# A gated recurrence and a two-layer network on one core: a plain first stretch, sums kept in PSUM, and another order of the blocks

## The chip, the cores and the metric

One Trainium2 chip, one of its cores. The time is device microseconds of one execution. Three runs of the kernel before gave 1103.45, 1106.84 and 1106.91 us, median 1106.84.

## The reference

Two parts follow each other. A recurrence along time, per batch and channel, and then a two-layer network with a gate on each of the 12,160 tokens, 256 channels wide with 2048 hidden values:

```
sig = 1 / (1 + exp(-f_logit))                 # (2, 6080, 256)
f = lower_bound + (1 - lower_bound) * sig
h = f[t] * h + (1 - f[t]) * x[t]              # for t in 0..6079, kept as token t
u = h @ w_in                                  # 256 x 2048
g = u * clip(u + 3, 0, 6) / 6
y = g @ w_out                                 # 2048 x 256
```

All inputs and outputs are float32.

## The kernel before

**Precision.** Every matrix operand is split in two: a rounded part ("hi", float32r) and what is left ("lo"). A product is three matmuls: hi*hi, hi*lo, lo*hi (L566, L568, L570 for the first layer, L587 to L589 for the second). ScalarE makes each hi part by a copy that rounds, VectorE or POOL makes the lo part by a subtraction.

**Tiles.** The 6080 time steps of each of the two batches are cut into a first span of 960 and five of 1024, which gives 12 tiles (t = 0 to 11; `TILES`), batches in turn. Within a tile, tokens are dealt in runs of four into two halves, FIRST and SECOND, so that a matmul has 480 columns in tiles 0 and 1 and 512 in the others.

**Seven products.** The first layer is a 2x2 block multiplication done with seven products instead of eight (Strassen's scheme in Winograd's form). Its operands are sums of quarters of the weights (`sum_w7`, POOL, once for each of the 8 blocks of 256 hidden values) and sums of quarters of the state (t_a, t_b, t_c; POOL, once per tile). The results are put together through running sums in a PSUM bank: `x_ps` takes A11, then S2, S1 and S4 on top of it, and between them ScalarE copies the state of the bank to `h_sb` (`copy_p1` L311, `copy_p16` L317, `copy_p165` L321). VectorE adds those copies to `z_ps` or `v_ps`: C11 (`add_c11`, L461), C22 (`add_c22`, L467), C21 (`add_c21`, L473). C12 is `x_ps` itself. C11, C22 and C21 are written to `h_sb`.

**A block** (q counts them, 96 in all; j is its number in the tile) has 7 products and 8 second-layer products ("downs", two for each of the four results), 45 matmuls. The downs are those of block q-1 and lie between the products of block q. For each result C: clip on ScalarE (`clip_lower`, L332), gate on VectorE (`gate_h`, L479), rounding on ScalarE (`round_g`, L339), rest on VectorE (`rest_of_g`, g_lo, L484), then the two downs.

**State of the next tile** is made during a tile: sigmoid on ScalarE (L282, blocks 2 and 3), then on VectorE drive (L426) and gate of the state (L432, a multiply and add with one input), and two scans (L440, L443), in blocks 2 to 5, always in front of the C11 sum; POOL and ScalarE then make the seven operands.

**Order.** Each engine has one queue, written out by hand, and runs it in order; the engines meet on semaphores. TensorE's order is in the loop at L600, ScalarE's at L363, VectorE's at L520, POOL's at L250, and SyncE issues all DMAs (L172 to L200). Before the first block, TensorE runs 36 small matmuls that only keep it busy, while VectorE, ScalarE and POOL make the state, operands and weights of block 0.

## Time and profile before

| What the page shows | |
|---|---|
| profiled execution | 1102.24 us, its span 1100.5 us |
| TensorE (PE) busy | 1018.1 us, 93% |
| VectorE (DVE) busy | 861.7 us, 78% |
| ScalarE (ACT) busy | 739.8 us, 67% |
| GpSimd (POOL) busy | 232.0 us, 21% |
| chain that ended last | DVE 35%, PE 30%, ACT 18%, issue 13% |
| L339 rounding, L332 clip of h_sb, mean | 617 ns, 720 ns |
| L317 copy of x_ps, mean | 584 ns |
| L479 gate, L484 g_lo, mean | 801 ns, 700 ns |
| L227 operand rest on POOL, mean | 1545 ns |
| x load of 512 KB, issue to landing | 7.1 us |
| mean granted clock of TensorE | 0.977 of full |

Busy time of TensorE counts overlapping matmuls once; a matmul's row lasts longer than the distance to the next one. So the rate is read from starts, and what is lost from the distance between equal places of two blocks or tiles. Idle time on an engine counts only where TensorE ends up waiting for it.

### The profile page before, as it was taken

The page shows a single profiled execution, that of the slowest core. Times are in us where ns is not written, and L with a number is a line of the kernel's source. Part 1 is how long each engine was busy: PE and PEld are TensorE (multiplying, and loading weights), DVE is VectorE, ACT ScalarE, POOL GpSimd, SP SyncE. Part 2 cuts the span into 40 slices and gives each one's busy share as a digit, 9 for nine tenths or more (in the row PEclk, how much of TensorE's full clock was granted, in tenths as well). Part 3 has the DMA queues.
Part 4 walks back from the last instruction along what each step waited for, and adds up shares of the span by engine and source line. Part 5 has one row for each costly group of instructions (what it writes and reads, how often), then busy time and mean ns, then how long its engine had stood idle before and what let it go on. Part 6 is the DMA issues. An engine that isn't in the chain of part 4 may idle for free.

```text
span 1100.5 us, 12941 instructions
## 1 busy us (share of the span) xinstructions
PE 1018.1 (93%) x4356; PEld 823.4 (75%) x4356; DVE 861.7 (78%) x1190; ACT 739.8 (67%) x1229; POOL 232.0 (21%) x176
## 2 busy tenths in 40 slices
PE   2788999998999999999899899999999999989998
PEld 2566787887777787787777778777778778777886
DVE  7687779788779778768778868877977886887675
ACT  3666676776776677676677677577767667766765
POOL 5655402202201301311210220220130121022000
PEclk7899999999999999999999999999999999999999
DMA  6200030030030030011003003003002000200000
GB/s 224 72 1 1 1 113 1 1 113 1 1 116 1 1 115 1 0 42 74 1 1 115 1 0 115 1 1 115 1 1 94 22 1 13 103 1 1 39 1 39
DMA packets 12707, 42.39 MB, mean 39 GB/s; under 512 B 1376, under 2 KB 1376, under 8 KB 12640
## 3 DMA queue, kind: packets, MB, share of 16 engines
q1 hardware_dynamic: 12640, 41.56, 10.4%
q8 instruction: 35, 0.57, 0.2%
q14 instruction: 32, 0.26, 0.1%
HBM read 29.10 MB, written 12.45 MB: 38 GB/s over the span
## 4 chain that ended last, share of the span: by engine, by line
DVE 35%; PE 30%; ACT 18%; issue 13%; DMA 2%; POOL 1%; SPq 0%; ACTq 0%; DVEq 0%; POOLq 0%
DVE g L479 14%; DVE g_lo L484 9%; ACT g_hi L339 8%; ACT g L332 6%; PE y_ps L587 5%; PE y_ps L588 5%; PE y_ps L589 5%; DVE h_sb L461 5%; PE x_ps L566 3%; PE x_ps L568 3%; PE x_ps L570 3%; DVE x_sb L426 3%; DVE x_sb L440 3%; DMA x_sb<-in_x 2%; PE v_ps L566 2%
## 5 line engine op out<-in xcount | busy, mean ns | idle before, releaser
L339 ACT CAST g_hi<-g 128x512 fp32r<-128x512 f32 (+1 forms) x384 | 233.9, 617 | 147.8 <-DVE g L479 146.3
L479 DVE SCALAR_TENSOR_TENSOR g<-g,h_sb 128x512 f32<-128x512 f32 (+1 forms) x288 | 230.6, 801 | 101.0 <-ACT g L332 99.0
L587 PE MATMUL y_ps<-g_hi,w_out_hi 128*128 128x512 f32 (+1 forms) x768 | 300.2, 391 | 0.3 <-DVE g_lo L484 0.3
L588 PE MATMUL y_ps<-g_lo,w_out_hi 128*128 128x512 f32 (+1 forms) x768 | 300.2, 391 | 0.0
L589 PE MATMUL y_ps<-g_hi,w_out_lo 128*128 128x512 f32 (+1 forms) x768 | 299.7, 390 | 0.0
L332 ACT ACTIVATE g<-h_sb,half 128x512 f32<-128x512 f32 (+1 forms) x288 | 207.4, 720 | 128.0 <-DVE h_sb L461 126.4
L484 DVE TENSOR_TENSOR g_lo<-g,g_hi 128x512 fp32r<-128x512 f32 (+1 forms) x384 | 261.2, 700 | 38.6 <-ACT g_hi L339 15.0
L566 PE MATMUL x_ps<-op_hi,w_hi 128*128 128x512 f32 (+1 forms) x384 | 154.2, 402 | 36.8 <-ACT h_sb L311 25.0
L587 PEld LDWEIGHTS y_ps<-g_hi,w_out_hi 128*128 128x128 f32 x768 | 145.5, 190 | 30.7 <-DVE g_lo L484 0.8
L589 PEld LDWEIGHTS y_ps<-g_hi,w_out_lo 128*128 128x128 f32 x768 | 145.7, 190 | 29.5
L588 PEld LDWEIGHTS y_ps<-g_lo,w_out_hi 128*128 128x128 f32 x768 | 145.5, 189 | 29.6
L568 PE MATMUL x_ps<-op_lo,w_hi 128*128 128x512 f32 (+1 forms) x384 | 151.3, 394 | 0.0
L570 PE MATMUL x_ps<-op_hi,w_lo 128*128 128x512 f32 (+1 forms) x384 | 150.6, 392 | 0.0
L566 PEld LDWEIGHTS x_ps<-op_hi,w_hi 128*128 128x128 f32 x384 | 73.6, 192 | 60.7 <-ACT h_sb L311 33.3
L566 PE MATMUL v_ps<-op_hi,w_hi 128*128 128x512 f32 (+1 forms) x192 | 81.8, 426 | 40.0 <-DVE h_sb L467 39.4
L461 DVE TENSOR_TENSOR h_sb<-z_ps,h_sb 128x512 f32<-128x512 f32 (+1 forms) x96 | 64.9, 676 | 66.3 <-PE z_ps L570 66.3
L236 POOL TENSOR_TENSOR t_a<-x_sb 128x512 f32<-128x512 f32 (+1 forms) x12 | 16.1, 1338 | 362.9 <-DVE x_sb L443 362.9
L317 ACT COPY h_sb<-x_ps 128x512 f32<-128x512 f32 (+1 forms) x96 | 56.0, 584 | 47.8 <-PE x_ps L570 47.5
L566 PEld LDWEIGHTS v_ps<-op_hi,w_hi 128*128 128x128 f32 x192 | 36.7, 191 | 67.6 <-DVE h_sb L467 62.2
L570 PEld LDWEIGHTS x_ps<-op_hi,w_lo 128*128 128x128 f32 x384 | 73.7, 192 | 15.1
L568 PEld LDWEIGHTS x_ps<-op_lo,w_hi 128*128 128x128 f32 x384 | 73.8, 192 | 14.1
L227 POOL TENSOR_TENSOR op_lo<-x_sb,op_hi 128x512 fp32r<-128x512 f32 (+1 forms) x34 | 52.1, 1545 | 148.7 <-ACT op_hi L307 148.7
(64 smaller groups left out, 1202.1 us busy)
## 6 DMA issues: line engine op xcount, KB each, us to landing
z_sb<-in_z SPq DMA_DIRECT2D x20, 512.0 KB, 6.2
x_sb<-in_x SPq DMA_DIRECT2D x20, 512.0 KB, 7.1
out_y<-y_sb SPq DMA_DIRECT2D x9, 1024.0 KB, 5.3
w_raw<-in_w_in SPq DMA_DIRECT2D x8, 256.0 KB, 7.5
w_out_raw<-in_w_out SPq DMA_DIRECT2D x8, 256.0 KB, 7.5
z_sb<-in_z SPq DMA_DIRECT2D x4, 480.0 KB, 4.4
x_sb<-in_x SPq DMA_DIRECT2D x4, 480.0 KB, 5.6
out_y<-y_sb SPq DMA_DIRECT2D x2, 960.0 KB, 5.3
```

Source lines behind the costliest of these rows:

```text
L317: nc.scalar.copy(h_sb[:, C21, 0:n], x_ps[:, q % 2, 0:n]).then_inc(p16_copied, 1)
L332: nc.scalar.activation(g[:, u, 0:n], h, ACT.Relu, bias=half[:], scale=1.0 / 6.0).then_inc(clipped_ready[u], 1)
L339: nc.scalar.copy(g_hi[:, u, 0:n], g[:, u, 0:n]).then_inc(g_hi_ready[u], 1)
L461: nc.vector.tensor_tensor(h_sb[:, C11, 0:n], z_ps[:, 0:n], h_sb[:, C11, 0:n], ALU.add).then_inc(h_ready[C11], 1)
L479: nc.vector.scalar_tensor_tensor(g[:, u, 0:n], g[:, u, 0:n], 1.0, h, ALU.min, ALU.mult).then_inc(g_ready[u], 1)
L484: nc.vector.tensor_tensor(g_lo[:, u, 0:n], g[:, u, 0:n], g_hi[:, u, 0:n].bitcast(F32), ALU.subtract).then_inc(g_lo_ready[u], 1)
L566: nc.tensor.matmul(out[:, 0:n], w7_hi[:, j, o], op_hi[:, b, o, 0:n], start=start, stop=False, skip_group_check=True)
L568: nc.tensor.matmul(out[:, 0:n], w7_hi[:, j, o], op_lo[:, b, o, 0:n], start=False, stop=False, skip_group_check=True)
L570: return nc.tensor.matmul(out[:, 0:n], w7_lo[:, j, o], op_hi[:, b, o, 0:n], start=False, stop=True, skip_group_check=True)
L587: nc.tensor.matmul(out, w_out_hi[:, f, at], g_hi[:, u, 0:n], start=opens, stop=False)
L588: nc.tensor.matmul(out, w_out_hi[:, f, at], g_lo[:, u, 0:n], start=False, stop=False)
L589: return nc.tensor.matmul(out, w_out_lo[:, f, at], g_hi[:, u, 0:n], start=False, stop=closes)
```

## The change

It has three parts.

**1. The first 960 tokens (batch 0) are worked plainly,** with the weights as they are, not with seven products. This "head" is in two parts of 448 and 512 tokens, 16 units of 128 hidden values each (32 units, v = 0 to 31). A unit is two first-layer products and two downs, 12 matmuls; four units are in flight (`LEAD`), in the four banks `x_ps` (2), `z_ps`, `v_ps`. The clip and the gate read the bank directly. Only 11 seven-product tiles are left (88 blocks), of which the first has 480 columns. The plain weights are rounded and their rests made one block at a time in the head's units; the sums for the seven products are made on POOL in three groups during the head (`sum_weights`, `make_s3`), S3's last, since its place holds a weight that the head still reads. State and operands of tile 0 are made in units 13 to 31. Warm-up matmuls: 28 instead of 36.

**2. Sums in place.** C11 is added into `z_ps` and C21 into `v_ps`; clip and gate read them there. C22 stays in `h_sb`.

**3. A new order in the blocks.** TensorE: both C22 downs before S1; S4 between the C21 downs, in front of A22. ScalarE: C12 is clipped before C21, and roundings of C12 and C21 move behind the next block's `copy_p1`. VectorE: the next tile's work stands behind the last gate of a block; rest_of_g for C21 and C12 moves around the next C11 sum. The gate of the state moves from VectorE to ScalarE (`make_gate`, an ACTIVATE with scale and bias). Scans for channel half 0 come in blocks 0 and 1, for half 1 in blocks 3 and 4, one per block; drives in blocks 7 and 2. SyncE loads z as soon as the scan has read it, two tiles ahead, and x when its sums are made.

```diff
-WARM_UP = 36
+WARM_UP = 28
+LEAD = 4
...
-    TILES = STEPS * B
+    TILES = STEPS * B - 1
+    HEAD_AT = (0, FIRST_SPAN - N)
+    HEAD_N = (FIRST_SPAN - N, N)
+    HEAD = len(HEAD_N) * F
+    GROUPS = (slice(0, 2), slice(2, 5), slice(5, 8))
...
 @block.gpsimd
+            def make_s3(i):
+                at = GROUPS[i]
+                raw = raw_of(at)
+                pool.wait_ge(head_up_done, F + 2 * at.stop)
+                nc.gpsimd.tensor_tensor(w7_raw[:, at, S3_T3], raw[:, :, 0], raw[:, :, 2],
+                                        ALU.subtract).then_inc(w_s3_ready, 1)
...
 @block.scalar
+            def make_gate(t, k):
+                n = 2 * half_span(t)
+                act.wait_ge(drive_ready[k], t + 1)
+                nc.scalar.activation(z_sb[:, k, 0:n], z_sb[:, k, 0:n], ACT.Identity, bias=one[:],
+                                     scale=lb_minus_one[:, k:k + 1]).then_inc(gate_ready[k], 1)
...
+            def head_clip(v):
+                s, n = v % LEAD, HEAD_N[v // F]
+                act.wait_ge(head_up_done, v + 1)
+                if v >= LEAD:
+                    act.wait_ge(head_g_lo_ready, v - LEAD + 1)
+                nc.scalar.activation(g[:, s, 0:n], head_bank(s, n), ACT.Relu, bias=half[:],
+                                     scale=1.0 / 6.0).then_inc(head_clipped_ready, 1)
...
 @block.vector
             def add_c11(q, n):
-                nc.vector.tensor_tensor(h_sb[:, C11, 0:n], z_ps[:, 0:n], h_sb[:, C11, 0:n],
+                nc.vector.tensor_tensor(z_ps[:, 0:n], z_ps[:, 0:n], h_sb[:, C11, 0:n],
                                         ALU.add).then_inc(h_ready[C11], 1)
...
             def add_c21(q, n):
-                nc.vector.tensor_tensor(h_sb[:, C21, 0:n], v_ps[:, 0:n], h_sb[:, C21, 0:n],
+                nc.vector.tensor_tensor(v_ps[:, 0:n], v_ps[:, 0:n], h_sb[:, C21, 0:n],
                                         ALU.add).then_inc(h_ready[C21], 1)
...
 @block.tensor
+            for v in range(LEAD, HEAD):
+                for d in range(K):
+                    head_down(v - LEAD, d)
+                for k in range(K):
+                    up = head_up(v, k)
+                up.then_inc(head_up_done, 1)
...
                 product(q, A12_B21, z_ps, True, n).then_inc(p2_ready, 1)
-                if q > 0:
-                    down(q - 1, C22, 0)
+                before(q, C22, 0)
+                before(q, C22, 1)
                 pe.wait_ge(p16_copied, q + 1)
                 product(q, S1_T1, bank, False, n).then_inc(p165_ready, 1)
-                if q > 0:
-                    pe.wait_ge(h_ready[C21], q)
+                if q == 0:
+                    pe.wait_ge(head_g_ready, HEAD)
+                else:
+                    pe.wait_ge(g_ready[C21], q)
                 product(q, S3_T3, v_ps, True, n).then_inc(p7_ready, 1)
-                if q > 0:
-                    down(q - 1, C22, 1).then_inc(down_done[C22], 1)
-                    down(q - 1, C21, 0)
+                before(q, C21, 0)
+                pe.wait_ge(p165_copied, q + 1)
+                product(q, S4_B22, bank, False, n).then_inc(c12_ready, 1)
+                before(q, C21, 1)
                 pe.wait_ge(h_ready[C22], q + 1)
                 product(q, A22_T4, v_ps, False, n).then_inc(p74_ready, 1)
```

TensorE's queue of a middle tile, before: from the end of product S3 (the first row) to product A22. The numbers in the semaphores' names are 0 for C11, 1 for C22, 2 for C21, 3 for C12.

```order
L570 MATMUL v_ps<-op_hi,w7_lo 128x512
L587 MATMUL y_ps<-g_hi,w_out_hi 128x512 [waits g_lo_ready1]
L588 MATMUL y_ps<-g_lo,w_out_hi 128x512
L589 MATMUL y_ps<-g_hi,w_out_lo 128x512
L587 MATMUL y_ps<-g_hi,w_out_hi 128x512 [waits g_lo_ready2]
L588 MATMUL y_ps<-g_lo,w_out_hi 128x512
L589 MATMUL y_ps<-g_hi,w_out_lo 128x512
L566 MATMUL v_ps<-op_hi,w7_hi 128x512 [waits h_ready1]
L568 MATMUL v_ps<-op_lo,w7_hi 128x512
L570 MATMUL v_ps<-op_hi,w7_lo 128x512
```

After, from the same place:

```order
L931 MATMUL v_ps<-op_hi_odd,w7_lo 128x512
L947 MATMUL y_ps<-g_hi,w_out_hi 128x512 [waits g_lo_ready2]
L948 MATMUL y_ps<-g_lo,w_out_hi 128x512
L949 MATMUL y_ps<-g_hi,w_out_lo 128x512
L929 MATMUL x_ps<-op_hi_odd_top,w7_hi 128x512 [waits p165_copied]
L930 MATMUL x_ps<-op_lo_odd_top,w7_hi 128x512
L931 MATMUL x_ps<-op_hi_odd_top,w7_lo 128x512
L947 MATMUL y_ps<-g_hi,w_out_hi 128x512 [waits g_lo_ready2]
L948 MATMUL y_ps<-g_lo,w_out_hi 128x512
L949 MATMUL y_ps<-g_hi,w_out_lo 128x512
L929 MATMUL v_ps<-op_hi_odd,w7_hi 128x512 [waits h_ready1]
```

S4 (x_ps) and a second C21 down now stand where a C22 down stood, so three products lie between S3 and the wait for the C22 sum (h_ready1), where two did.

VectorE's queue of a middle tile, before: blocks 4 and 5 begin with the work for the next tile, in front of the C11 sum (L461).

```order
L426 SCALAR_TENSOR_TENSOR x_sb<-z_sb,one_minus_lb,x_sb 128x1024 [waits x_loaded1,sig_ready1]
L432 TENSOR_SCALAR z_sb<-z_sb,lb_minus_one 128x1024 [waits drive_ready1]
L461 TENSOR_TENSOR h_sb<-z_ps,h_sb 128x512 [waits p1_copied,p2_ready]
L479 SCALAR_TENSOR_TENSOR g<-g,h_sb 128x512 [waits clipped_ready0]
L467 TENSOR_TENSOR h_sb<-v_ps,h_sb 128x512 [waits p165_copied,p7_ready]
L484 TENSOR_TENSOR g_lo<-g,g_hi 128x512 [waits g_hi_ready0]
L479 SCALAR_TENSOR_TENSOR g<-g,h_sb 128x512 [waits clipped_ready1]
L473 TENSOR_TENSOR h_sb<-v_ps,h_sb 128x512 [waits p16_copied,p74_ready]
```

After, from the last gate of a block (L727 with v_ps), a scan, and the begin of the next:

```order
L727 SCALAR_TENSOR_TENSOR g<-g,v_ps 128x512 [waits clipped_ready2]
L699 SCALAR_TENSOR_TENSOR x_sb<-z_sb,carry,x_sb 128x512 [waits carry_ready,gate_ready0]
L732 TENSOR_TENSOR g_lo<-g,g_hi 128x512 [waits g_hi_ready2]
L710 TENSOR_TENSOR z_ps<-z_ps,h_sb 128x512 [waits p1_copied,p2_ready]
L732 TENSOR_TENSOR g_lo<-g,g_hi 128x512 [waits g_hi_ready3]
L727 SCALAR_TENSOR_TENSOR g<-g,z_ps 128x512 [waits clipped_ready0]
L716 TENSOR_TENSOR h_sb<-v_ps,h_sb 128x512 [waits p165_copied,p7_ready]
L732 TENSOR_TENSOR g_lo<-g,g_hi 128x512 [waits g_hi_ready0]
L727 SCALAR_TENSOR_TENSOR g<-g,h_sb 128x512 [waits clipped_ready1]
```

The scan (L699) stands behind the gates. The subtractions g_lo (L732) of the block before lie on both sides of the C11 sum (L710), which now writes z_ps. The state's gate (L432) has left this queue.

ScalarE's queue, before: end of block 0 of a tile, begin of block 1. L346 copies y of the tile before.

```order
L332 ACTIVATE g<-h_sb,half 128x512 [waits g_lo_ready1,h_ready1]
L339 CAST g_hi<-g 128x512 [waits down_done1,g_ready1]
L346 COPY y_sb<-y_ps 128x128x4 [waits y_stored,down_done2] x2
L332 ACTIVATE g<-h_sb,half 128x512 [waits g_lo_ready2,h_ready2]
L332 ACTIVATE g<-x_ps,half 128x512 [waits g_lo_ready3,c12_ready]
L311 COPY h_sb<-x_ps 128x512 [waits p1_ready]
L346 COPY y_sb<-y_ps 128x128x4 [waits y_stored,down_done3]
L339 CAST g_hi<-g 128x512 [waits down_done2,g_ready2]
L339 CAST g_hi<-g 128x512 [waits down_done3,g_ready3]
L317 COPY h_sb<-x_ps 128x512 [waits g_ready2,p16_ready]
L346 COPY y_sb<-y_ps 128x128x4 [waits y_stored,down_done3]
```

After:

```order
L473 ACTIVATE z_sb<-z_sb,one,lb_minus_one 128x1024 [waits drive_ready0]
L518 COPY y_sb<-y_ps 128x128x4 [waits y_stored,down_done2]
L499 ACTIVATE g<-x_ps,half 128x512 [waits g_lo_ready3,c12_ready]
L508 CAST g_hi<-g 128x512 [waits down_done1,g_ready1]
L518 COPY y_sb<-y_ps 128x128x4 [waits y_stored,down_done2]
L499 ACTIVATE g<-v_ps,half 128x512 [waits g_lo_ready2,h_ready2]
L478 COPY h_sb<-x_ps 128x512 [waits p1_ready]
L508 CAST g_hi<-g 128x512 [waits down_done3,g_ready3]
L508 CAST g_hi<-g 128x512 [waits down_done2,g_ready2]
L518 COPY y_sb<-y_ps 128x128x4 [waits y_stored,down_done3]
L484 COPY h_sb<-x_ps 128x512 [waits h_ready2,p16_ready]
L518 COPY y_sb<-y_ps 128x128x4 [waits y_stored,down_done3]
```

Between the clip of C22 and the clip of C21 (v_ps) of block 0 there are now the state's gate and two y copies, and in block 1 the two roundings stand in front of the y copy that waits for down_done3.

## Rows read from the trace of the kernel before

**Rows 1.** Busy time by window; columns: window, its length, each engine, clock, DMA
```profile
0.00:28.00 28.00, 8.20 (x39) 7.27 (x39) 20.62 (x23) 9.82 (x14) 16.66 (x18) 0.73 0.62 220
28.00:130.10 102.10, 84.06 (x342) 67.95 (x342) 78.98 (x97) 63.65 (x110) 60.92 (x49) 0.92 0.06 20
130.10:212.80 82.70, 79.63 (x362) 67.03 (x360) 66.56 (x99) 58.49 (x103) 16.34 (x11) 1.00 0.11 38
212.80:1009.80 797.00, 760.29 (x3241) 610.90 (x3240) 636.39 (x883) 549.98 (x910) 138.05 (x99) 0.99 0.10 36
```

**Rows 2.** Timeline, last tile, TensorE; columns: start us, length us, engine, line, operation
```profile
1069.75 0.39 PE L566 MATMUL x_ps<-op_hi,w_hi 128*128 128x512 f32 x1
...
1079.95 0.39 PE L566 MATMUL x_ps<-op_hi,w_hi 128*128 128x512 f32 x1
```

**Rows 3.** Timeline, TensorE, 480 columns
```profile
35.08 0.38 PE L566 MATMUL x_ps<-op_hi,w_hi 128*128 128x480 f32 x1
...
35.73 0.38 PE L566 MATMUL x_ps<-op_hi,w_hi 128*128 128x480 f32 x1
```

**Rows 4.** Timeline, ScalarE: the first copy of tiles 1, 2 and 11
```profile
130.15 0.55 ACT L311 COPY h_sb<-x_ps 128x480 f32<-128x480 f32 x1
...
212.75 0.58 ACT L311 COPY h_sb<-x_ps 128x512 f32<-128x512 f32 x1
...
1009.82 0.58 ACT L311 COPY h_sb<-x_ps 128x512 f32<-128x512 f32 x1
```

**Rows 5.** Waits from 212.8 to 1009.8; columns: us in total, times, longest
```profile
PEld v_ps L566 <- DVE h_sb L467: 52.6, 45, 2.6
```

**Rows 6.** Timeline, VectorE, blocks 4 and 5 of a middle tile
```profile
608.87 1.28 DVE L426 SCALAR_TENSOR_TENSOR x_sb<-z_sb,one_minus_lb,x_sb 128x1024 f32<-128x1024 f32 x1
610.19 1.66 DVE L432 TENSOR_SCALAR z_sb<-z_sb,lb_minus_one 128x1024 f32<-128x1024 f32 x1
611.77 0.68 DVE L461 TENSOR_TENSOR h_sb<-z_ps,h_sb 128x512 f32<-128x512 f32 x1
613.24 0.69 DVE L479 SCALAR_TENSOR_TENSOR g<-g,h_sb 128x512 f32<-128x512 f32 x1 [0.79 <-ACT g L332]
613.85 0.68 DVE L467 TENSOR_TENSOR h_sb<-v_ps,h_sb 128x512 f32<-128x512 f32 x1
...
621.32 2.13 DVE L443 TENSOR_TENSOR_SCAN x_sb<-z_sb,x_sb 128x512 f32<-128x512 f32 x1
623.37 0.66 DVE L461 TENSOR_TENSOR h_sb<-z_ps,h_sb 128x512 f32<-128x512 f32 x1
624.82 1.77 DVE L479 SCALAR_TENSOR_TENSOR g<-g,h_sb 128x512 f32<-128x512 f32 x1 [0.79 <-ACT g L332]
```

**Rows 7.** Timeline, TensorE and ScalarE, the same blocks
```profile
609.49 0.39 PE L570 MATMUL x_ps<-op_hi,w_lo 128*128 128x512 f32 x1
...
609.91 0.59 ACT L317 COPY h_sb<-x_ps 128x512 f32<-128x512 f32 x1 [0.68 <-PE x_ps L570]
...
614.59 0.50 PE L566 MATMUL v_ps<-op_hi,w_hi 128*128 128x512 f32 x1 [0.63 <-DVE h_sb L467]
```

**Rows 8.** Timeline, POOL, the same tile
```profile
624.77 1.27 POOL L265 TENSOR_TENSOR t_c<-x_sb 128x512 f32<-128x512 f32 x1
```

**Rows 9.** Groups, 212.8 to 1009.8; columns: count, busy us, mean ns, idle before
```profile
L479 DVE SCALAR_TENSOR_TENSOR g<-g,h_sb 128x512 f32<-128x512 f32 x216 | 170.7, 790 | 71.5 <-ACT g L332 69.9
...
L479 DVE SCALAR_TENSOR_TENSOR g<-g,x_ps 128x512 f32<-128x512 f32 x72 | 49.0, 681 | 4.8 <-ACT g L332 4.8
...
L282 ACT ACTIVATE z_sb<-z_sb 128x1024 f32<-128x1024 f32 x18 | 19.1, 1061 | 0.0
```

**Rows 10.** Timeline, the start: first sigmoid, first drive, second product
```profile
4.36 1.00 ACT L282 ACTIVATE z_sb<-z_sb 128x960 f32<-128x960 f32 x1 [2.34 <-DMA z_sb<-in_z]
...
7.09 1.22 DVE L426 SCALAR_TENSOR_TENSOR x_sb<-z_sb,one_minus_lb,x_sb 128x960 f32<-128x960 f32 x1 [2.31 <-DMA x_sb<-in_x]
...
28.63 0.77 PE L566 MATMUL x_ps<-op_hi,w_hi 128*128 128x480 f32 x1 [8.35 <-ACT h_sb L311]
```

807 lines of the change are left out of this document (561 added, 246 removed).

## The prediction

> **What bounds the kernel now.** I read the stages first [rows 1]. TensorE is busy for 95 or 96% of both windows between 130 and 1010 us, so the reader should see a kernel near its matmul rate, with a poor start and a small leak everywhere else. How fast it could go stands in the last tile, which prepares no next tile: two starts of the first product of a block lie 1079.95 - 1069.75 = 10.20 us apart, 45 matmuls of 512 columns at 0.2267 us each [rows 2]. At 480 columns three matmuls take 35.73 - 35.08 = 0.65 us, so one is 0.2167 and a block 9.75 us [rows 3]. (A row's own duration, 0.39, overlaps its neighbours; starts count.)
>
> Against that rate the stages lose this. The copy that follows the first product of a tile marks the tiles [rows 4]. Up to 130.15 us one tile is done whose matmuls need 78.0: 52 us lost. Tile 1 takes 82.6 for 78.0. From 212.75 to 1009.82 nine tiles take 797.1 us, 88.56 each, against 8 x 10.20 = 81.6: 63 us lost. Of the waits in that stretch the weight load in front of the second v_ps product is the large one, 52.6 us over 45 waits, always for the C22 sum on VectorE (L467) [rows 5].
>
> Why that sum is late is in VectorE's order of time [rows 6]. From the C11 sum (611.77) to the C11 gate (613.24) pass 1.47 us, because ScalarE's clip lies between; the C22 sum starts 0.61 later, and TensorE starts its product right at its end, 614.59, after 0.63 us idle [rows 7]. In front of the C11 sum stand drives, gates and scans. A second effect sits in the same rows: the scan took 2.13 and a gate with both inputs in SBUF 1.77, while a sum with a PSUM input in the same neighbourhood took 0.66. POOL was working then [rows 8]. Over the stretch the gate with h_sb averages 790 ns, the one with x_ps 681 [rows 9].
>
> [...]
>
> **Steady tiles, step by step.** I put a block's time zero at its first product and each product at 0.68 us (3 x 0.2267). Order now: A11 0, C11 downs, S2 2.04, A12 2.72, C22 downs, S1 4.76, S3 5.44, C21 down, S4 6.80, C21 down, A22 8.16, C12 downs, end 10.20. A result can be read 0.42 us after its last matmul starts (609.49 to 609.91) [rows 7], so z_ps at 3.6, v_ps after S3 at 6.3.
> - C22 sum: before, its consumer A22 came 1.36 us after S3, now 2.04 after it, and S3 itself comes 0.68 later after A12. From the C11 sum's start to the C22 sum's end pass at least 1.47 + 0.61 + 0.68 = 2.76 us. Before, A22 wanted it 3.2 after z_ps: 0.4 us room. Now it wants it at 8.16, 4.56 after z_ps: 1.8 us room, 1.2 once v_ps decides (6.3 + 0.68).
> - The new tight place is S4 behind copy_p165, which is queued on ScalarE behind the C11 clip: sum 3.6 to 4.3, clip to 5.0, copy to 6.2, wanted 6.80. The sum may be 1.2 us late.
> - VectorE's load per block [rows 6, 9]: 3 sums at 0.68, 4 gates at 0.68, 4 g_lo at 0.69 (the small table has 0.70 as the mean over all), plus per tile two drives and four scans at 1.28 (the two gate instructions, 1.66 beside POOL, leave): 7.5 + 0.96 = 8.5 us of 10.20. At most one 1.28 piece falls into one block, and behind the last gate; before it was two (608.87 to 611.77) in front of the C11 sum [rows 6]. Lateness is made good within the block.
> - The C11, C21 and head gates now read PSUM, so they fall to 0.68 even beside POOL. The two sums written into PSUM have no row. Lower bound: 0.66, the shortest sum. Upper bound: the longest row of rows 6 at 512 columns but the scan, 1.77. I take 0.68, the row it is nearest to (same instruction, same inputs).
> - ScalarE per block (the small table's means): 3 copies at 0.58, 4 roundings at 0.62, clips at 0.67 from PSUM: 6.95; per tile 2 sigmoids and now 2 gates at 1.06, 7 operand roundings, 4 y copies: 1.37 per block, 8.3 together. The gate on ScalarE has no row; it is the same ACTIVATE at the same 1024 columns as the sigmoid, 1.06 [rows 9]; bounds 0.72, the mean clip of half the columns, and twice that, 1.45 (0.8 us more per tile, 8 in all).
> - Where ScalarE is too full: block 0 of a tile, gate and two y copies between clip C22 and clip C21. Clip C21 ends near 12.0 instead of 10.6, so the next copy_p1 ends at 12.5 and S2 wants it at 12.24; then two roundings stand in front of the y copy for the SECOND half, C22's first down waits for it 0.3, its second 0.4. Loss about 1.3 us per tile. Queued behind: everything on ScalarE, but the blocks 2 to 7 have room. I add 0.3 per tile for scans beside POOL.
> - SyncE's queue: z is now loaded as soon as the state is scanned, x once POOL has made t_c (near block 6), and the y store stands behind both. x lands 7.1 us after its issue (small table), the drive comes at the end of block 7, some 10 us later: nothing, and if the cover went, one drive late by the difference, absorbed as above.
> So a tile takes 81.6 + 1.6 = 83.2 (bounds 81.8 and 86.0), nine of them 748.8 against 797.1.
>
> **The head.** It has 384 matmuls for 960 tokens, 24 more than the 360 of the seven-product way: 192 of 448 columns (0.203 each, an estimate on the line through rows 2 and 3) and 192 of 512 (0.2267).
> - Start: z and x come in 448 columns instead of 960. Before, the sigmoid starts at 4.36 and the drive at 7.09 [rows 10]; the drive should now start near 5.3. Drive 0.6, gate 0.4, scan 1.2, w_lo 0.7, operand rest 0.6: first product near 9 us. The second channel, with scans as long as the 2.13 of 621.32 [rows 6], gives 13 to 14; clip, gate, rounding and g_lo of the first unit let the first down start near 17. The kernel before reaches its second product at 28.63 [rows 10].
> - From there 336 matmuls up to the first seven-product block (four units' downs lie in that block): 168 x 0.203 + 168 x 0.2267 = 72.2, to 89.
> - Is TensorE the slowest there? Per unit it needs 2.4 to 2.7 us. VectorE: gate and g_lo 1.3, 32 units 42; g_lo beside POOL 0.35 more (estimate between 0 and 1.08), 11; five w_lo, head gates, scans and the next tile's state work 18: 71 us in 72. It is level. From a product's end to its down 7.1 us pass and the chain needs 5, so 2 us of lateness are hidden. ScalarE waits in its queue for POOL's weight sums and t_c near the end; clips behind it are 1 to 3 us late. I charge 6 us for all this and for a TensorE at the lower clock after the idle start (a mean of 0.73 in the first window [rows 1], which lies between the two levels, 2.4 GHz and half of it): first block at 95.
> - Eight warm-up matmuls fewer, all of them over before 9 us either way: nothing.
> - The weights' sums are hidden: S3's sum waits for the head's products up to unit 20, is needed at 100.
> - First seven-product tile: 8 x 9.75 + 1.4 = 79.4, so 1920 tokens are done at 174.4. Before it was 212.75 - 0.87 = 211.9. Gain 37.5.
>
> **Sum.** 174.4 + 748.8 = 923.2. The last tile and its tail took 1100.5 - 1008.95 = 91.55; I add the 1.3 of the tile boundary and 1.4 because g_lo of C21, wanted second by the last downs, is now made last: 94.3. Span 1017.5. The profiled execution was 1102.24 for a span of 1100.5, so 1019.2; the median of the runs lay 0.4% over the profiled one, of which I take half: 1021 us.
>
> **Rivals.**
> - Steady tiles stay held by ScalarE: its queue gains two gates, and if every block, not only block 0, loses 0.55 us, a tile takes 86.0: 28 us more, 1049. For it: 8.3 of 10.2 busy and in-order waits. Against it: no other block has three extra pieces, and the clips wait less than before (L332 for L461 loses a scan in front).
> - The head is held by VectorE: if each of 32 g_lo pays the full 1.08, it has 94 us of work for 72, less what POOL's pauses and the charged 6 give back: 14 more, 1035. [...]
> - No boundary loss and a clean head: 16 + 5 less, 1000.
> - Slower: the sums written in place. Two per block, 88 blocks. VectorE has 10.2 - 8.5 = 1.7 us room, less 0.3 for POOL; once a sum costs more than 0.7 extra, VectorE sets the block, and each further 0.1 us costs 17.6 us. 86 us are eaten at 0.7 + 0.49 = 1.2 us extra, a sum of 1.88 us instead of 0.68. At 2.0 us the time is 1128. Against it: no 512-column row is that long, and PSUM reads are not dear.
> The Trainium skill, "VectorE: DVE Perf Modes", section The TRN2 errata, gives VectorE 120 fixed cycles from PSUM against 58 from SBUF, 65 ns more; the trace disagrees (681 ns with x_ps [rows 9], 0.69 with h_sb where POOL rested, at 613.24 [rows 6]). Even doubled in both sums it would be an estimate of 0.26 us per block, inside the room.
> - The change not doing what it says: the order of instructions shows the new order on TensorE and the gates on ScalarE, so none.
>
> **From this the numbers.** Forecast (1002 to 1035) 0.68, ScalarE 0.12, VectorE in the head 0.10, clean 0.05, in-place sums dear 0.05, of which 0.04 slower and 0.01 even. A difference within 0.3% can't be told from none. Low 1000, high 1052.
>
> **What would show it.** Right: blocks of 10.2 us in tiles 1 to 9 save for the first two; the wait of v_ps on L716 nearly gone; the sums L710 and L722 at 0.68; first head product near 9 us, first seven-product block near 95. Wrong: L710 over 1.0 us; S4 waiting for copy_p165 in every block; gaps of TensorE behind g_lo in the head of over 0.5 us per unit.

## The result, and the profile after

The changed kernel takes 1013.84 us, the median of 4 runs (1013.15 to 1014.54), beside 1105.14 us, the median of 4 runs of the kernel before on the same chip. The ratio is 0.9176, 95% interval 0.9152 to 0.92. The forecast was 1021 us in a range of 1000 to 1052. The profiled execution took 1013.79 us, its span 1011.6.

The chain that ended last, by engine. Before, its shares were 35% on VectorE and 30% on TensorE.

```profile
PE 87%; DVE 4%; issue 3%; ACT 3%; POOL 1%; DMA 0%; SPq 0%; ACTq 0%; DVEq 0%; POOLq 0%
```

Busy time by window after the change, for [rows 1] (columns as there). The windows are: the start, the head's first units, the rest of the head, the first seven-product tile, the nine middle tiles, the last tile. The bounds at 96.40, 175.50 and 918.30 lie 0.9 us before the copies that mark the tiles.

```profile
0.00:17.00 17.00, 12.74 (x52) 10.99 (x52) 9.37 (x17) 7.39 (x13) 4.21 (x7) 0.90 0.88 296
17.00:42.50 25.50, 24.45 (x120) 21.99 (x119) 24.44 (x34) 18.26 (x33) 10.84 (x6) 1.00 0.29 97
42.50:96.40 53.90, 51.76 (x229) 42.33 (x227) 44.92 (x50) 37.03 (x61) 40.66 (x28) 1.00 0.18 60
96.40:175.50 79.10, 77.06 (x351) 65.62 (x352) 64.61 (x95) 58.02 (x103) 20.66 (x14) 1.00 0.11 34
175.50:918.30 742.80, 741.33 (x3241) 606.11 (x3240) 602.66 (x865) 550.54 (x926) 144.94 (x99) 1.00 0.11 36
918.30:1011.60 93.30, 87.66 (x385) 71.74 (x383) 60.30 (x93) 58.82 (x99) 0.00 (x0) 0.99 0.06 23
```

TensorE is busy for 741.3 of 742.8 us in the middle tiles, where it was 760.3 of 797.0 [rows 1]. The copy that marks the tiles [rows 4] is now L478 (timeline, ScalarE; the first copies of the first and second seven-product tile and of the last):

```profile
97.32 0.56 ACT L478 COPY h_sb<-x_ps 128x480 f32<-128x480 f32 x1
...
176.42 0.59 ACT L478 COPY h_sb<-x_ps 128x512 f32<-128x512 f32 x1 [0.64 <-PE x_ps L931]
...
919.21 0.59 ACT L478 COPY h_sb<-x_ps 128x512 f32<-128x512 f32 x1 [0.30 <-PE x_ps L931]
```

So 1920 tokens are done 36.3 us earlier (212.75 - 176.42). The nine middle tiles take 742.8 us for 797.1, 82.5 each for 88.6: 54.3 us less. The last tile with its tail is 1.8 us longer. Together 88.8, which is the difference of the spans, 1100.5 - 1011.6 = 88.9.

The waits of TensorE's weight loads from 177 to 918 us, for [rows 5]:

```profile
PEld y_ps L947 <- ACT y_sb L518: 6.6, 18, 0.5
PEld x_ps L929 <- ACT h_sb L478: 5.2, 9, 0.6
```

The wait for the C22 sum, 52.6 us before, is gone. What is left comes at the boundary of each tile: one wait for `copy_p1` and two for the y copies. The groups of VectorE in the whole page of the profile (columns: count, busy us, mean ns, idle before), for [rows 9]:

```profile
L716 DVE TENSOR_TENSOR h_sb<-v_ps,h_sb 128x512 f32<-128x512 f32 (+1 forms) x88 | 60.5, 688 | 43.4 <-PE v_ps L931 43.2
...
L710 DVE TENSOR_TENSOR z_ps<-z_ps,h_sb 128x512 f32<-128x512 f32 (+1 forms) x88 | 60.9, 693 | 17.0 <-PE z_ps L931 17.0
...
L727 DVE SCALAR_TENSOR_TENSOR g<-g,v_ps 128x512 f32<-128x512 f32 (+1 forms) x88 | 60.2, 684 | 14.7 <-ACT g L499 14.7
L727 DVE SCALAR_TENSOR_TENSOR g<-g,h_sb 128x512 f32<-128x512 f32 (+1 forms) x88 | 60.5, 687 | 11.7 <-ACT g L499 11.0
```

A sum written into PSUM costs 693 ns, one written into SBUF 688. The gates with h_sb no longer average 790 ns: three of the four gates read PSUM, and the fourth (C22, with h_sb) now falls where POOL rests, in 87 of its 88 instances.

### The profile page after: what moved, and what is told of

Its sections match the earlier page's. It is cut to its first block, busy times and chain, and to the rows that moved or that the text cites. A ratio compares the mean times of both kernels' runs of the same rounds, so it can differ in the third digit from the quotient of the medians.

```text
span 1011.6 us, 12907 instructions
## 1 busy us (share of the span) xinstructions
PE 995.0 (98%) x4372; PEld 818.8 (81%) x4372; DVE 806.3 (80%) x1149; ACT 730.1 (72%) x1230; POOL 221.3 (22%) x154
## 4 chain that ended last, share of the span: by engine, by line
PE 87%; DVE 4%; issue 3%; ACT 3%; POOL 1%; DMA 0%; SPq 0%; ACTq 0%; DVEq 0%; POOLq 0%
PE y_ps L947 15%; PE y_ps L948 14%; PE y_ps L949 14%; PE x_ps L929 8%; PE x_ps L930 7%; PE x_ps L931 7%; PE v_ps L931 4%; PE v_ps L930 4%; PE v_ps L929 4%; PE z_ps L929 2%; PE z_ps L930 2%; PE z_ps L931 2%; PE y_ps L911 1%; PE y_ps L913 1%; PE y_ps L912 1%
## 5 line engine op out<-in xcount | busy, mean ns | idle before, releaser
L732 DVE TENSOR_TENSOR g_lo<-g,g_hi 128x512 fp32r<-128x512 f32 (+1 forms) x352 | 271.1, 770 | 42.1 <-ACT g_hi L508 41.3
L508 ACT CAST g_hi<-g 128x512 fp32r<-128x512 f32 (+1 forms) x352 | 209.1, 620 | 14.4 <-DVE g L727 13.7
L499 ACT ACTIVATE g<-v_ps,half 128x512 f32<-128x512 f32 (+1 forms) x88 | 60.5, 687 | 58.3 <-DVE v_ps L722 58.3
L499 ACT ACTIVATE g<-z_ps,half 128x512 f32<-128x512 f32 (+1 forms) x88 | 60.4, 687 | 57.5 <-DVE z_ps L710 56.3
L716 DVE TENSOR_TENSOR h_sb<-v_ps,h_sb 128x512 f32<-128x512 f32 (+1 forms) x88 | 60.5, 688 | 43.4 <-PE v_ps L931 43.2
L727 DVE SCALAR_TENSOR_TENSOR g<-g,x_ps 128x512 f32<-128x512 f32 (+1 forms) x88 | 59.8, 680 | 40.1 <-ACT g L499 40.1
L499 ACT ACTIVATE g<-h_sb,half 128x512 f32<-128x512 f32 (+1 forms) x88 | 63.6, 723 | 24.0 <-DVE h_sb L716 23.7
L929 PE MATMUL x_ps<-op_hi_even,w_hi 128*128 128x512 f32 (+1 forms) x192 | 75.2, 391 | 2.7 <-ACT h_sb L478 2.3
L710 DVE TENSOR_TENSOR z_ps<-z_ps,h_sb 128x512 f32<-128x512 f32 (+1 forms) x88 | 60.9, 693 | 17.0 <-PE z_ps L931 17.0
L930 PE MATMUL x_ps<-op_lo_even,w_hi 128*128 128x512 f32 (+1 forms) x192 | 74.5, 388 | 0.0
L931 PE MATMUL x_ps<-op_hi_even,w_lo 128*128 128x512 f32 (+1 forms) x192 | 74.4, 388 | 0.0
L727 DVE SCALAR_TENSOR_TENSOR g<-g,v_ps 128x512 f32<-128x512 f32 (+1 forms) x88 | 60.2, 684 | 14.7 <-ACT g L499 14.7
L727 DVE SCALAR_TENSOR_TENSOR g<-g,h_sb 128x512 f32<-128x512 f32 (+1 forms) x88 | 60.5, 687 | 11.7 <-ACT g L499 11.0
L478 ACT COPY h_sb<-x_ps 128x512 f32<-128x512 f32 (+1 forms) x88 | 51.2, 581 | 25.7 <-PE x_ps L931 25.7
```

The source lines that it names most:

```text
L499: nc.scalar.activation(g[:, u, 0:n], up_result(q, u, n), ACT.Relu, bias=half[:], scale=1.0 / 6.0).then_inc(clipped_ready[u], 1)
L508: nc.scalar.copy(g_hi[:, u, 0:n], g[:, u, 0:n]).then_inc(g_hi_ready[u], 1)
L710: nc.vector.tensor_tensor(z_ps[:, 0:n], z_ps[:, 0:n], h_sb[:, C11, 0:n], ALU.add).then_inc(h_ready[C11], 1)
L716: nc.vector.tensor_tensor(h_sb[:, C22, 0:n], v_ps[:, 0:n], h_sb[:, C22, 0:n], ALU.add).then_inc(h_ready[C22], 1)
L727: nc.vector.scalar_tensor_tensor(g[:, u, 0:n], g[:, u, 0:n], 1.0, up_result(q, u, n), ALU.min, ALU.mult).then_inc(g_ready[u], 1)
L732: nc.vector.tensor_tensor(g_lo[:, u, 0:n], g[:, u, 0:n], g_hi[:, u, 0:n].bitcast(F32), ALU.subtract).then_inc(g_lo_ready[u], 1)
```

## The experiments

The trace says where the time went, not which part of the change brought it. Two parts aim at the same wait: the new order gives the C22 sum more room, and the sums in place keep the work in front of it short. All times are medians of 4 runs. They come from different chips, so the ratio, to the kernel before on the same chip, is the safer number to compare. "A tile" is the mean of the nine middle tiles between the marks above, from the one traced execution of each kernel; for the kernel before it is 88.56 us.

| Kernel | us | ratio, 95% interval | a tile, us |
|---|---|---|---|
| changed kernel | 1013.84 | 0.9176 [0.9152, 0.9200] | 82.53 |
| e1_sums_sbuf | 1017.08 | 0.9219 [0.9196, 0.9242] | 82.71 |
| e2_gate_dve | 1010.97 | 0.9165 [0.9143, 0.9186] | 81.68 |
| e3_pe_order | 1135.55 | 1.0297 [1.0267, 1.0327] | 90.80 |
| e4_pe_order_back | 1004.79 | 0.9111 [0.9089, 0.9133] | 81.59 |
| h1_sbuf_old_order | 1026.81 | 0.9300 [0.9286, 0.9314] | 83.69 |
| h2_in_place | 1063.34 | 0.9631 [0.9615, 0.9647] | 85.04 |
| h3_in_place_gate | 1064.90 | 0.9644 [0.9626, 0.9661] | 85.22 |
| g1_paired | 1005.11 | 0.9103 [0.9087, 0.9119] | 81.65 |
| g2_round_end | 1012.21 | 0.9170 [0.9150, 0.9190] | 82.55 |
| g4_all_back | 1035.70 | 0.9385 [0.9366, 0.9404] | 84.53 |
| g3_no_head | 1036.53 | 0.9390 [0.9371, 0.9410] | 82.52 |
| h4_best | 1003.68 | 0.9095 [0.9079, 0.9110] | 81.59 |

**e1_sums_sbuf: the sums out of PSUM again.** Changed kernel, and:

```diff
-                nc.vector.tensor_tensor(z_ps[:, 0:n], z_ps[:, 0:n], h_sb[:, C11, 0:n],
+                nc.vector.tensor_tensor(h_sb[:, C11, 0:n], z_ps[:, 0:n], h_sb[:, C11, 0:n],
...
-                nc.vector.tensor_tensor(v_ps[:, 0:n], v_ps[:, 0:n], h_sb[:, C21, 0:n],
+                nc.vector.tensor_tensor(h_sb[:, C21, 0:n], v_ps[:, 0:n], h_sb[:, C21, 0:n],
```

> The changed kernel with one part undone: the C11 and C21 sums go to SBUF (h_sb) again, and their gates read them there, so they have two SBUF inputs. Theory (room in the order carries the gain): the gates beside POOL cost up to 1.08 us more, 0.11 us on average over all, but 1.2 us of room take nearly all of it: 1014 to 1019 us, the gate L727 with h_sb near 0.79 mean, hardly a new wait on TensorE. Rival (sums in place are what removed the stalls): two contended gates per tile put about 1 us each on the path of ten tiles: 1032 us or more.

The time rose by 3.2 us, and the two intervals just touch. In the traces 1.8 us of the difference stand there before the first seven-product block has begun (its first copy at 99.16 for 97.32), where this edit changes nothing: TensorE was granted 0.84 of its clock in the first 17 us, where the changed kernel had 0.90. The middle tiles lose 0.18 us each, 1.6 in all. The gates with h_sb are slow again (VectorE's group of all three results that stand in SBUF, 177 to 910 us), yet TensorE waits 0.3 us in all for the C22 sum:

```profile
L723 DVE SCALAR_TENSOR_TENSOR g<-g,h_sb 128x512 f32<-128x512 f32 (+1 forms) x212 | 172.9, 815 | 27.7 <-ACT g L495 25.9
```

In the new order the sums in place are worth 2 to 3 us.

**e3_pe_order: TensorE's new order alone.** Kernel before, and in TensorE's loop:

```diff
-                    down(q - 1, C22, 0)
+                    down_both(q - 1, C22)
...
-                    down(q - 1, C22, 1).then_inc(down_done[C22], 1)
                     down(q - 1, C21, 0)
+                pe.wait_ge(p165_copied, q + 1)
+                product(q, S4_B22, bank, False, n).then_inc(c12_ready, 1)
+                if q > 0:
+                    down(q - 1, C21, 1).then_inc(down_done[C21], 1)
                 pe.wait_ge(h_ready[C22], q + 1)
                 product(q, A22_T4, v_ps, False, n).then_inc(p74_ready, 1)
-                if q > 0:
-                    down(q - 1, C21, 1).then_inc(down_done[C21], 1)
-                pe.wait_ge(p165_copied, q + 1)
-                product(q, S4_B22, bank, False, n).then_inc(c12_ready, 1)
```

> The kernel before with TensorE's new order alone (both C22 downs before S1, S4 and a C21 down between S3 and A22); ScalarE, VectorE and POOL as before. Theory (TensorE's order is the larger part of the steady gain): the wait for the C22 sum goes from 53 us to under 10, some comes back at C12 and C21, whose clips are in the old order; a tile falls from 88.6 to about 85.5, 1070 to 1080 us. Rival (what stands in front of the C11 sum on VectorE decides, the order only shifts who waits): 1095 or more.

It is 3% slower, where 1070 to 1080 us were expected. The waits of the weight loads from 212 to 1000 us:

```profile
PEld x_ps L566 <- ACT h_sb L311: 71.2, 60, 1.8
...
PEld v_ps L566 <- DVE h_sb L467: 5.7, 8, 0.7
```

The order does what I had computed for the C22 sum: 52.6 us of waiting become 5.7. But 71 us of another wait come in. The last tile, where no state work disturbs, shows the chain (timeline of VectorE, ScalarE, TensorE in turn):

```profile
1108.72 0.69 DVE L473 TENSOR_TENSOR h_sb<-v_ps,h_sb 128x512 f32<-128x512 f32 x1 [0.54 <-PE v_ps L570]
...
1109.44 0.72 ACT L332 ACTIVATE g<-h_sb,half 128x512 f32<-128x512 f32 x1 [0.61 <-DVE h_sb L473]
1110.07 0.67 ACT L332 ACTIVATE g<-x_ps,half 128x512 f32<-128x512 f32 x1
1110.93 1.22 ACT L339 CAST g_hi<-g 128x512 fp32r<-128x512 f32 x2 [0.18 <-DVE g L479]
1112.05 0.58 ACT L311 COPY h_sb<-x_ps 128x512 f32<-128x512 f32 x1
...
1112.68 0.50 PE L566 MATMUL x_ps<-op_hi,w_hi 128*128 128x512 f32 x1 [0.60 <-ACT h_sb L311]
```

A22 now ends later, so does the C21 sum. ScalarE, in its old order, clips C21 and C12 and rounds both before it copies the bank that S2 of the next block wants. Blocks 0 and 1 of a tile take 21.5 us together, and from block 2 on every block takes at least 11.09 us, in the last tile too, instead of 10.20. The changed kernel moves the roundings behind the copy, so it does not pay this; but the direction of the debt is shown: what the order gives the C22 sum it takes from the chain C21, ScalarE, `copy_p1`. The time lies where the rival had it (1095 or more), but that rival named VectorE's work in front of the C11 sum, and the wait that came in is one for ScalarE.

**e4_pe_order_back: everything but the order.** Changed kernel with the old order of products (shown), and C12's clip, gate and rounding behind C21's as before; the roundings stay behind `copy_p1`:

```diff
                 before(q, C22, 0)
-                before(q, C22, 1)
...
+                before(q, C22, 1)
                 before(q, C21, 0)
-                pe.wait_ge(p165_copied, q + 1)
-                product(q, S4_B22, bank, False, n).then_inc(c12_ready, 1)
-                before(q, C21, 1)
                 pe.wait_ge(h_ready[C22], q + 1)
                 product(q, A22_T4, v_ps, False, n).then_inc(p74_ready, 1)
+                before(q, C21, 1)
+                pe.wait_ge(p165_copied, q + 1)
+                product(q, S4_B22, bank, False, n).then_inc(c12_ready, 1)
```

> The changed kernel with the old order of products on TensorE (A22 before S4, one C22 down between S3 and it), and ScalarE's and VectorE's order of C12 and C21 turned back to match; head, sums in place and one piece of state work per block stay. Theory: room for the C22 sum falls to 0.4 us, every block with a drive or scan in front of it stalls 0.3 to 1 us: 3 us per tile, 1040 to 1050. Rival (order does not matter once VectorE has one piece per block): 1014 to 1020.

It is 9 us faster than the changed kernel (7 by the ratios, 8.5 in the middle tiles of the traces), below both the theory's range and the rival's. Between 175 and 910 us TensorE is never idle (busy time by window), and seven of the nine middle tiles are exactly 8 x 10.200 us:

```profile
175.00:910.00 735.00, 735.00 (x3245) 608.59 (x3243) 606.52 (x865) 552.49 (x925) 141.03 (x99) 1.00 0.11 36
```

The copy that is late in the changed kernel, the one of block 1 behind a tile's first block, is now in time: ScalarE reaches it 0.20 us before the product is done (timeline, ScalarE):

```profile
512.32 0.59 ACT L478 COPY h_sb<-x_ps 128x512 f32<-128x512 f32 x1 [0.20 <-PE x_ps L931]
```

My theory that the new product order is a main step of the gain falls here. In this kernel it is a loss. The edit takes the order of C12 and C21 on ScalarE and VectorE back with the products; the three were not separated.

**h1_sbuf_old_order: old order and sums in SBUF.** The kernel of e4 with the edit of e1.

> The changed kernel with the old order of products and of copies (as in e4_pe_order_back, 1004.79 us), and the sums of C11 and C21 written to SBUF again, nothing else. Theory: in the old order the sums in place are what carries the blocks, because with them the gates read PSUM and do not meet GpSimd's work; with the sums in SBUF the contended gates return and the matmuls of blocks 2, 5, 6 and 7 wait some 0.65 us each, 2.6 us per middle tile, nine tiles and a part of the last: 1025 to 1032 us. In the new order the same undoing cost 3.2 us. Rival: the old order has room enough by itself, since the state's gate is off VectorE: 1005 to 1010 us.

1026.81 us, 22 more than e4, as the theory had it. Middle tiles are 10.20 in blocks 0 to 4 and 11.03, 10.82 and 10.86 in blocks 5 to 7. The second row of the timeline (VectorE, then TensorE) is the C11 gate, 1.75 us with both inputs in SBUF beside POOL; the C22 sum stands behind it, and TensorE behind that:

```profile
566.66 0.69 DVE L706 TENSOR_TENSOR h_sb<-z_ps,h_sb 128x512 f32<-128x512 f32 x1
...
568.15 1.75 DVE L723 SCALAR_TENSOR_TENSOR g<-g,h_sb 128x512 f32<-128x512 f32 x1
569.83 0.68 DVE L712 TENSOR_TENSOR h_sb<-v_ps,h_sb 128x512 f32<-128x512 f32 x1
...
570.56 0.50 PE L925 MATMUL v_ps<-op_hi_odd,w_hi 128*128 128x512 f32 x1 [0.53 <-DVE h_sb L712]
```

POOL's work beside that gate:

```profile
566.16 3.19 POOL L352 TENSOR_TENSOR op_lo_even<-x_sb,op_hi_even 128x512 fp32r<-128x512 f32 x2 [0.20 <-ACT op_hi_even L464]
```

With e1 and e4 this closes a square. Old order: 1026.8 with the sums in SBUF, 1004.8 with the sums in place. New order: 1017.1 and 1013.8. Each of the two parts is a remedy for the same wait. The order gains 9.7 us where the sums are in SBUF and loses 9.1 where they are in place. The middle tiles of the traces say the same without the differences between chips and starts: 83.69 and 81.59 us in the old order, 82.71 and 82.53 in the new one.

**h2_in_place: the sums in place alone.** Kernel before with this part only (the clip and the gate read the bank; S3 waits for the gate of C21 in place of its sum):

```diff
-                nc.vector.tensor_tensor(h_sb[:, C11, 0:n], z_ps[:, 0:n], h_sb[:, C11, 0:n],
+                nc.vector.tensor_tensor(z_ps[:, 0:n], z_ps[:, 0:n], h_sb[:, C11, 0:n],
...
-                nc.vector.tensor_tensor(h_sb[:, C21, 0:n], v_ps[:, 0:n], h_sb[:, C21, 0:n],
+                nc.vector.tensor_tensor(v_ps[:, 0:n], v_ps[:, 0:n], h_sb[:, C21, 0:n],
...
-                    pe.wait_ge(h_ready[C21], q)
+                    pe.wait_ge(g_ready[C21], q)
```

> The kernel before with the sums of C11 and C21 left in place in PSUM, nothing else of the change. Theory: the sums in place alone take most of the stalls out of the blocks, some 3.5 us of the 5.9 to 7.3 us by which a tile of before is above its matmuls; ten tiles: 1065 to 1080 us. The blocks in which VectorE also holds the state's gate and drive keep a stall. Rival: the state's gate on VectorE and the order of TensorE set the stalls, and the sums alone give under 1 us per tile: 1098 us or more.

1063.34 us, 1.7 below the expected range: this part alone brings 41 us, 3.5 per middle tile (88.56 to 85.04) and 7.0 in the first two (212.75 to 205.78). It is the largest single part that I measured on the kernel before. About 8 of the 41 are the stretches at the lower clock in the middle tiles, which are not there any more (last section). What it leaves is the work in front of the C11 sum (timeline, VectorE, then TensorE):

```profile
577.81 1.28 DVE L448 TENSOR_TENSOR_SCAN x_sb<-z_sb,carry,x_sb 128x512 f32<-128x512 f32 x1
579.12 1.28 DVE L451 TENSOR_TENSOR_SCAN x_sb<-z_sb,x_sb 128x512 f32<-128x512 f32 x1
580.33 0.67 DVE L469 TENSOR_TENSOR z_ps<-z_ps,h_sb 128x512 f32<-128x512 f32 x1
...
583.10 0.50 PE L574 MATMUL v_ps<-op_hi,w_hi 128*128 128x512 f32 x1 [0.18 <-DVE h_sb L475]
```

**h3_in_place_gate: and the state's gate on ScalarE.** h2 with `make_gate` of the next tile behind C22's rounding on ScalarE in blocks 2 and 4:

```diff
+                    if j in (2, 4) and t + 1 < TILES:
+                        make_gate(t + 1, j // 2 - 1)
...
                             make_drive(t + 1, 0)
-                            make_gate(t + 1, 0)
...
                             make_drive(t + 1, 1)
-                            make_gate(t + 1, 1)
```

> The kernel of h2_in_place with the state's gate of every channel half moved from VectorE to ScalarE, and nothing else. Theory: VectorE has 1.66 us less to do in the blocks with state work, which is most of what h2 leaves: 10 to 15 us below h2, 1053 to 1068 us. Rival: with the sums in place VectorE has room already, and the gate's place does nothing: within 3 us of h2.

The rival is right: 1064.90 us, no different from h2. It lies in the theory's range too, but not 10 to 15 us below h2. The weight loads' wait for the C22 sum falls from 35.2 to 22.7 us (206 to 971 us), but a new one of 14.4 us for `copy_p1` (L327) takes its place, since the gate's 1.24 us stand in front of C21's clip (timeline, ScalarE, then TensorE):

```profile
574.56 1.24 ACT L322 ACTIVATE z_sb<-z_sb,one,lb_minus_one 128x1024 f32<-128x1024 f32 x1
575.71 0.66 ACT L347 ACTIVATE g<-v_ps,half 128x512 f32<-128x512 f32 x1
576.27 0.67 ACT L347 ACTIVATE g<-x_ps,half 128x512 f32<-128x512 f32 x1
577.12 1.22 ACT L354 CAST g_hi<-g 128x512 fp32r<-128x512 f32 x2 [0.18 <-DVE g L496]
578.25 0.58 ACT L327 COPY h_sb<-x_ps 128x512 f32<-128x512 f32 x1
...
578.88 0.50 PE L582 MATMUL x_ps<-op_hi,w_hi 128*128 128x512 f32 x1 [0.41 <-ACT h_sb L327]
```

**e2_gate_dve: the state's gate back on VectorE.** Changed kernel with `make_gate` on VectorE straight behind the drive:

```diff
+                dve.wait_ge(drive_ready[k], t + 1)
+                nc.vector.tensor_scalar(z_sb[:, k, 0:n], z_sb[:, k, 0:n], lb_minus_one[:, k:k + 1], 1.0,
+                                        ALU.mult, ALU.add).then_inc(gate_ready[k], 1)
```

> The changed kernel with the state's gate back on VectorE, right behind the drive, instead of on ScalarE. Theory (the loss at the tile boundary, blocks 0 and 3, is ScalarE's queue with the gate in it): blocks 0 and 3 fall to 10.2 us, which gives 1.2 us per tile, 12 in all; drive and gate together (1.28 + 0.75 to 1.66) make the next C11 sum about 1 us late, within the room of 1.2 or just over it, at most 0.5 us twice per tile: 1004 to 1012, I take 1007. Rival (VectorE needed the relief): the C11 sum comes too late in blocks 0 and 3, over 1 us each: 1025 or more.

1010.97 us. The intervals of the ratios overlap with those of the changed kernel, so the times alone decide nothing; the traces do. A middle tile is 81.68 us instead of 82.53: without the gate in block 0, ScalarE's `copy_p1` is in time. Nine tiles give back 7.7 us, and the first seven-product block starts 4.5 us later (its copy at 101.78 for 97.32). Of these, 1.6 are there at the first down already (19.87 for 18.32), with the longer lower clock of e1's start (0.84 granted over the first 17 us). Then TensorE's two waits for g_lo in the head grow from 2.0 to 4.8 us, since VectorE has the gates of the state in its queue.

**g1_paired, g2_round_end, g4_all_back: the rest of the block's layout,** each on the kernel of e4. g1 puts both scans of a channel half into one block, still behind the last gate (shown for half 1; half 0 likewise, in block 1):

```diff
-                    if j == 3:
-                        scan(t + 1, 1, FIRST)
                     if j == 4:
+                        scan(t + 1, 1, FIRST)
                         scan(t + 1, 1, SECOND)
```

> The version with the old product order (1004.8 us) with the two scans of a channel half in one block again (blocks 1 and 4), still behind the last gate. Theory now (what stands in front of the C11 sum decides, room 0.4 us): one scan ends 1.5 us after the block's start, two end at 2.8 to 3.6, with a g_lo behind them the C11 sum starts up to 0.7 us late: 0 to 0.5 us twice per tile, 1005 to 1013 us. Rival (pairing is the main cause of the 7 us per tile before): 1030 or more.

1005.11 us, the same as e4. Whether a block has one scan or two does not matter here, once they stand behind the last gate. In g2 the roundings of C21 and C12 and their rests stand at the block's end again, ahead of `copy_p1`:

```diff
                 clip_lower(q, C12, n)
+                round_g(q, C21, n)
+                round_g(q, C12, n)
...
                 gate_h(q, C12, n)
+                rest_of_g(q, C21, n)
+                rest_of_g(q, C12, n)
```

> The version with the old product order (1004.8 us) with the roundings of C12 and C21 at the end of the block again, in front of copy_p1, and both g_lo behind the last gate, so in front of the state work. Theory (VectorE's load in front of the C11 sum): the roundings fill ScalarE's 1.3 us of idle time, both g_lo end 2.1 us after the block's start, a scan behind them at 3.4, before z_ps is ready at 3.6: 1005 to 1010. Rival (the place of the roundings is what freed the blocks): copy_p1 or the C11 sum comes over 0.4 us late in most blocks, 1030 or more.

1012.21 us: 7.4 more than e4, above the theory's range and far below the rival's. It is 0.96 per middle tile, and block 0 alone is 1.1 us longer (11.29), where the state's gate and the y copies are too. g4 is e4 with paired scans, the state's gate on VectorE and the sums in SBUF:

> The version with the old product order (1004.8 us) with three things turned back together: scans in pairs, the state's gate on VectorE behind the drive, and the C11 and C21 sums in SBUF. Theory (VectorE's work in front of the C11 sum, with what POOL adds to it): drives with gates and paired scans meet contended gates of 1.3 to 1.8 us; a tile takes 84 to 87 us instead of 81.6, 1030 to 1055. Rival (the roundings' place alone keeps the blocks free, whatever the load): under 1015.

1035.70 us, 9 more than h1, which has only the sums in SBUF. Where VectorE has room (e4), paired scans cost nothing; where the contended gates have used it up, paired scans and the gate on VectorE together cost 0.84 us per middle tile. The gate on VectorE also delays the first seven-product block, as in e2 (its copy at 99.89 for h1's 97.13).

**g3_no_head: the start of before with the changed blocks.** Twelve seven-product tiles, no plain first 960 tokens; blocks as in the changed kernel.

> The kernel before with the whole block part of the change (sums in place, product order, roundings, one piece of state work per block, gate on ScalarE, early z loads), but without the head: 12 seven-product tiles and the old start. Theory (head and blocks add up): the head gave 36.4 us (175.5 against 211.9 at the end of 1920 tokens), so this lies 30 to 38 us over the changed kernel: 1045 to 1052. Rival (the new blocks also mend the first tile, and the head adds little): 1030 or less.

1036.53 us, 22.7 more than the changed kernel, less than the theory's 30 and more than the rival allowed. Its tiles 0 and 1 take 92.4 and 78.9 us where before had 102.1 and 82.6. So of the 36.3 us gained over the first 1920 tokens 14.1 come from the new blocks (212.75 - 198.69, its mark of tile 2) and 22.3 from the head (198.69 - 176.42). Head and blocks do add up, but both work on the first tiles, and the head is worth less than the 36.4 us that I had put down to it. What within the head brings the 22 us (shorter first loads, less work before the first product) was not separated.

**h4_best.** e4 with C21's last rounding (shown) and rest ahead of C12's:

```diff
-            round_g(LAST, C12, half_span(TILES - 1))
             round_g(LAST, C21, half_span(TILES - 1))
+            round_g(LAST, C12, half_span(TILES - 1))
```

> The kernel of e4_pe_order_back with one more edit: in the last block alone ScalarE rounds C21 and g_lo ahead of C12, so that the last down products start earlier. Theory: only the work behind the last block's products is shorter, some 1.5 us: 1003.3 us, 1002.5 to 1004.5. Rival: the last products are held by something else (g_hi's gate on VectorE), and the time stays at 1004.8 us.

1003.68 us, ratio 0.9095 for e4's 0.9111: the intervals overlap. In the traces the stretch from the last tile's mark to the end is 91.0 us for 92.2. This kernel has the lowest median of all, 1.0% below the changed one, though it can't be told from e4 by the times.

## Why the prediction came out, and where it was wrong

The time was forecast 0.7% too high, inside the range. By the terms of the sum: 1920 tokens were done at 175.5 us, forecast 174.4; the nine middle tiles took 742.8, forecast 748.8; the last tile with its tail took 93.3, forecast 94.3; and the 2 us added because the median had lain over the profiled execution were not there (1013.84 and 1013.79). For my reason for the gain in the middle tiles the near miss is luck: the forecast starts from TensorE's own rate and adds a loss at the boundary, so it would have been the same number whichever part of the change had freed the blocks. By its own steps:

- **Matmul rate, 10.20 us per block: right.** The kernel of e4 runs at this through nine tiles (81.59 us each for 8 x 10.20).
- **Head: right.** First product at 9.35 (forecast 9), the second channel's at 14.68 (13 to 14), first down at 18.32 (17), first product of the first seven-product block at 94.14 (95). From the first down to there 75.8 us passed, 72.2 of them matmuls. The second product of that block then stood 1.6 us idle for `copy_p1`, behind ScalarE's last work for the head, so 5.2 of the 6 us that I had charged were spent. But the prediction credited the whole gain over the first 1920 tokens, 37.5 us, to its account of the head; by g3 the head's share is 22.3, and the new blocks bring 14.1. The rows (timeline, TensorE), for [rows 10]:

```profile
9.35 0.44 PE L899 MATMUL x_ps<-op_hi_odd,w_hi 128*128 128x448 f32 x1 [2.01 <-DVE op_lo_odd L776]
...
14.68 0.44 PE L899 MATMUL x_ps<-op_hi_odd,w_hi 128*128 128x448 f32 x1 [1.07 <-DVE op_lo_odd L776]
18.32 0.44 PE L911 MATMUL y_ps<-g_hi,w_out_hi 128*128 128x448 f32 x1 [0.97 <-DVE g_lo L795]
...
94.14 0.38 PE L929 MATMUL x_ps<-op_hi_even,w_hi 128*128 128x480 f32 x1
...
97.93 0.49 PE L929 MATMUL x_ps<-op_hi_even,w_hi 128*128 128x480 f32 x1 [1.58 <-ACT h_sb L478]
```

- **g_lo beside POOL, 0.35 us more in the head: right,** 1036 ns on average from 17 to 96.4 us:

```profile
L795 DVE TENSOR_TENSOR g_lo<-g,g_hi 128x448 fp32r<-128x448 f32 (+1 forms) x31 | 32.1, 1036 | 0.1
```

 VectorE was nevertheless hardly what held the head: TensorE was busy for 76.2 of 79.4 us there, and waited for g_lo twice behind the first down, 2.0 us in all. What interference with POOL's work costs is shown by the gate: 1.75 us in h1 with both inputs in SBUF, 0.68 to 0.69 from PSUM. The Trainium skill, "SBUF — State Buffer", section Who interferes with whom, states that a VectorE instruction with two SBUF inputs contends with a GpSimd instruction that reads SBUF, and that one with at most one SBUF input does not, outside the modes that use both ports; the gate agrees. The number of SBUF inputs alone does not decide it: the state's gate on VectorE has one and took 1.66 us beside POOL, 0.75 without it, and the page counts its kind of instruction, tensor_scalar, among those that can enter such a mode.
- **Sums written to PSUM at 0.68 us: right** (693 ns), so the slower rival had nothing to stand on. Its "no 512-column row is that long" was wrong as a reading: the scan in [rows 6] is one, with 2.13 us.
- **The state's gate on ScalarE at 1.06 us: mis-sized,** it is 1.23, inside the bounds of 0.72 and 1.45.
- **Loss at the tile boundary of 1.3 + 0.3 us: the place was right, the size 0.93.** This is where the 6.0 us of the middle tiles went. The terms listed for the boundary, 0.26, 0.3 and 0.4, add up to 0.96 and not to 1.3. And the 0.3 for scans beside POOL had nothing behind it: all 36 scans of the middle tiles took 1.28 us. The timeline around 517 us shows what I had described: gate, y copy and y copy in front of the clip of C21, `copy_p1` behind it, the stalled S2, and then two y copies that TensorE's downs wait for. S2 starts at 518.10 behind a matmul at 517.57, 0.30 us late. (ScalarE, then TensorE, with the last waits.)

```profile
513.24 1.23 ACT L473 ACTIVATE z_sb<-z_sb,one,lb_minus_one 128x1024 f32<-128x1024 f32 x1
...
515.92 0.59 ACT L518 COPY y_sb<-y_ps 128x512 f32<-128x512 f32 x1
...
516.88 0.69 ACT L499 ACTIVATE g<-v_ps,half 128x512 f32<-128x512 f32 x1 [0.37 <-DVE v_ps L722]
...
517.47 0.58 ACT L478 COPY h_sb<-x_ps 128x512 f32<-128x512 f32 x1
...
518.10 0.50 PE L929 MATMUL x_ps<-op_hi_odd_top,w_hi 128*128 128x512 f32 x1
...
519.62 0.19 PEld L947 LDWEIGHTS y_ps<-g_hi,w_out_hi 128*128 128x128 f32 x1 [0.30 <-ACT y_sb L518]
```

- **"C22 sum: ... Now it wants it at 8.16 ... 1.8 us room": the step that was wrong in its weight.** The room is there, and e3 shows it working (52.6 us of waiting become 5.7). But I made it the reason for the gain in the middle tiles, and gave the sums in place only a clause. e4 shows that no more room is needed than the old 0.4 us, once the C11 gate reads PSUM and the next tile's work stands behind the last gate. And the same step should have been worked out for what moves the other way: A22 comes 1.36 us later, so do the C21 sum and its clip, and `copy_p1` behind them. I had seen the late `copy_p1` behind block 0 and put it down to the gate and the y copies alone; with both still there, but without the new order, that copy is in time, by 0.20 us (e4).
- **The boundary's cause is therefore two things together, and either undone removes it:** the old order (e4: 81.59) or the gate off ScalarE (e2: 81.68). The roundings in front of the copy bring it back in the old order (g2: 82.55), so ScalarE's whole load there counts.
- **The tail's 1.4 us for g_lo of C21 made last: about right.** h4 undoes it in e4 and the stretch from the last mark falls by 1.2 us.

The 91 us, as far as the runs separate them: the head 22 to 23; the sums in place 41 when they come first, 2 to 3 when they come last; the new order +33 us alone, -10 and +9 in the square above. Between h2's tile (85.04) and e4's (81.59) lie the place of the next tile's work, of the roundings and of the state's gate, and the earlier loads. The gate's place brought nothing in h3. The roundings are 0.96 (g2, measured from e4). The earlier loads were not run alone, but in the kernel before VectorE waited for an x load only twice in nine tiles, 2.7 us in all. Moving the state work behind the last gate was not run alone on the kernel before; that it is the rest is argued from h2's rows, not shown.

## What to carry to other kernels

When a change holds two remedies for one wait, run the four combinations: a remedy that gains alone may cost once the other is in. When a step is moved to give one result more room, work out in the same table what the moved-back results now do to the queues that serve them. And an operation with both inputs in SBUF on VectorE beside GpSimd's work is worth moving onto a PSUM operand, which need not cost anything itself.

## What the hardware showed that I had not expected

- **A stall of TensorE was sometimes followed by the lower clock.** In six of the nine middle tiles of before, the longest wait for the C22 sum was followed at once by 3.4 us at the lower of the two levels (1.2 GHz instead of 2.4), and block 5 took 14.0 us instead of 12.66: 1.35 us each, 8 us in all. Rows of before, timeline of VectorE and TensorE:

```profile
443.55 2.13 DVE L443 TENSOR_TENSOR_SCAN x_sb<-z_sb,x_sb 128x512 f32<-128x512 f32 x1
...
447.06 1.77 DVE L479 SCALAR_TENSOR_TENSOR g<-g,h_sb 128x512 f32<-128x512 f32 x1 [0.79 <-ACT g L332]
448.75 0.68 DVE L467 TENSOR_TENSOR h_sb<-v_ps,h_sb 128x512 f32<-128x512 f32 x1
...
449.48 0.69 PE L566 MATMUL v_ps<-op_hi,w_hi 128*128 128x512 f32 x1 [2.12 <-DVE h_sb L467]
```

 And busy time by window around that start (the last three columns: granted clock, DMA share, GB/s):

```profile
448.00:449.60 1.60, 0.12 (x1) 0.12 (x2) 1.51 (x3) 0.74 (x2) 0.27 (x1) 1.00 0.00 0
449.60:453.00 3.40, 3.40 (x9) 2.66 (x10) 3.04 (x5) 1.92 (x3) 0.00 (x0) 0.50 0.00 0
```

 The same wait of 2.12 us at 361.91 was followed by none. In all nine tiles that wait was 2.12 to 2.17 us long, so its length does not tell the six from the three. After the change, and in h2, no such dip comes in the middle tiles.
- **A VectorE sum with a PSUM operand that writes PSUM** took 693 ns on average (512 columns, a few of 480), 5 ns more than one that writes SBUF.
- **The same multiply and add of 1024 columns** took 1.23 us on ScalarE, and on VectorE 0.75 (h2 at 568.97) or 1.66 beside POOL (before at 610.19 [rows 6]).
